# A fused attention and two-MLP kernel: nine slots with two MLP units, a third raw weight buffer, and another release for the low halves

## The reference

```python
scores = scale * q @ k.T                       # per batch and head, 576 x 576
kth = 32nd largest of each row
attn = softmax(where(scores >= kth, scores, -1e9))
x = attn @ v                                   # (4, 576, 512)
u = x + real(fft(fft(x, axis=1), axis=2))      # over tokens, then over width
u = u + relu(norm(u) @ w_ch1) @ w_ch2          # first MLP, norm without gain
out = u + relu((norm(u) * g_ln) @ w_ch1b) @ w_ch2b   # second MLP
```

## Time and profile before

| | us |
|---|---|
| median of 3 runs | 1462.12 |
| lowest to highest | 1460.74 to 1468.54 |
| the profiled execution | 1469.69 |
| its span, first to last instruction | 1467.9 |
| PE busy | 1299.5 (89%) |
| DVE busy | 1173.1 (80%) |
| ACT busy | 765.2 (52%) |
| POOL busy | 339.4 (23%) |

### The profile page before, as it was taken

The page is one execution under the profiler, slowest core; times in us unless marked ns, Lnnn a source line. Parts: engine busy times, 40 slices in busy tenths (PEclk is TensorE's granted clock), DMA queues, the critical chain, the costliest instruction groups (busy, mean ns, idle before and its releaser), DMA issues.

```text
span 1467.9 us, 22757 instructions
## 1 busy us (share of the span) xinstructions
PE 1299.5 (89%) x7944; PEld 1050.6 (72%) x7944; DVE 1173.1 (80%) x2332; ACT 765.2 (52%) x1480; POOL 339.4 (23%) x296
## 2 busy tenths in 40 slices
PE   4777778799989789778989988989999999999999
PEld 2444444577767677667877767877788999989898
DVE  8999999779999998899898899953675454555554
ACT  4666664466666554465563555542345344444433
POOL 3433330112122251122152132230113030121210
PEclk7878778899999889899998989999999999999999
DMA  6888892365646655666664656632344343333342
GB/s 228 292 308 311 290 341 88 131 230 197 225 155 218 228 193 177 218 219 224 240 204 152 214 199 221 215 127 98 101 158 158 129 138 128 126 119 125 119 149 82
DMA packets 113939, 274.34 MB, mean 187 GB/s; under 512 B 29345, under 2 KB 29346, under 8 KB 113826
## 3 DMA queue, kind: packets, MB, share of 16 engines
q1 hardware_dynamic: 102066, 225.68, 44.9%
q10 hardware_dynamic: 10368, 42.47, 8.3%
q0 software_dynamic: 1392, 4.73, 1.0%
HBM read 229.58 MB, written 42.73 MB: 186 GB/s over the span
## 4 chain that ended last, share of the span: by engine, by line
PE 51%; DVE 31%; DMA 6%; issue 5%; ACT 3%; POOL 3%; SPq 0%; ACTq 0%; DVEq 0%; POOLq 0%
PE Big L695 21%; DVE top L1041 13%; DVE wk L1053 12%; PE Big L678 11%; PE Sp L678 7%; DMA wf<-in_weights 6%; DVE ex L1060 3%; PE Tp L649 2%; PE Sp L722 2%; PE Tp L626 2%; DVE nmx L1048 2%; PE Sp L734 1%; PE Tp L643 1%; POOL un L497 1%; PE Tp L753 1%
## 5 line engine op out<-in xcount | busy, mean ns | idle before, releaser
L695 PE MATMUL Big<-wr,hh 128*128 128x512 f32 x1152 | 366.6, 400 | 0.0
L678 PE MATMUL Big<-uh,wr 128*128 128x256 f32 (+1 forms) x1336 | 305.9, 319 | 19.0 <-ACT hh L910 17.2
L1041 DVE MAX8 top<-wk 128x8 f32<-128x576 f32 x432 | 304.2, 744 | 0.0
L678 PEld LDWEIGHTS Big<-uh,wr 128*128 128x128 f32 x1336 | 225.8, 193 | 39.7 <-issue 29.1
L695 PEld LDWEIGHTS Big<-wr,hh 128*128 128x128 f32 x1152 | 220.5, 191 | 42.3
L695 PE MATMUL Big<-wr,hl 128*128 128x512 f32 x576 | 240.3, 417 | 4.6 <-DVE wr L1192 4.4
L1053 DVE MATCH_REPLACE8 wk<-top,wk 128x576 f32<-128x576 f32 x288 | 211.3, 740 | 0.0
L462 POOL TENSOR_TENSOR hl<-hf,hh 128x256 fp32r<-128x256 f32 (+1 forms) x111 | 93.3, 841 | 505.8 <-ACT hh L910 505.8
L678 PE MATMUL Big<-ul,wr 128*128 128x256 f32 (+1 forms) x668 | 208.3, 312 | 0.0
L626 PE MATMUL Tp<-ident,ex 128*128 128x128 f32 x720 | 121.6, 299 | 63.9 <-DVE ex L1060 59.7
L626 PEld LDWEIGHTS Tp<-ident,ex 128*128 128x128 f32 x720 | 90.0, 151 | 110.2 <-issue 78.2
(11 more groups left out here) (134 smaller groups left out, 1944.0 us busy)
## 6 DMA issues: line engine op xcount, KB each, us to landing
wf<-in_weights SPq DMA_DIRECT2D x200, 512.0 KB, 4.3
wr<-w_low SPq DMA_DIRECT2D x222, 256.0 KB, 4.1
sc<-in_weights SPq DMA_DIRECT2D x56, 512.0 KB, 3.2
sc<-sc_ahead ACTq DMA_DIRECT2D x36, 576.0 KB, 5.8
w_low<-wr SPq DMA_DIRECT2D x32, 512.0 KB, 6.8
sc_ahead<-U ACTq DMA_DIRECT2D x18, 576.0 KB, 5.5
sc_ahead<-un ACTq DMA_DIRECT2D x9, 576.0 KB, 3.1
sc_ahead<-yb ACTq DMA_DIRECT2D x9, 576.0 KB, 6.4
```

Of the source, the lines that this page charges most:

```text
L678: last = nc.tensor.matmul(hidden(n), a[:, kd * P:(kd + 1) * P], x[:, kd, 0:P * SIZE[p]], start=(kd == 0 and j == 0), stop=(kd == KD - 1 an ...
L695: last = nc.tensor.matmul(Ac[:, j, :], a[:, n % 2, j * P:(j + 1) * P], w, start=(f == 0 and m == 0), stop=(f == KF - 1 and m == 2))
L1041: nc.vector.max(top[:, s % RING, r, :], src).then_inc(s_top, 1)
```

## The change

- `DOUBLE` names nine slots (86, 92, 98, 104, 110, 121, 126, 132, 138) which carry two units. `UP` becomes 120, the list ends at slot 249, and the groups from the fifth on start earlier: 95, 109, 123, 137, 152, 168, ... in place of 97, 113, 129, 145, 161, 177, ...
- In such a slot the second unit stands last: PE runs its first layer and the first unit's second layer after `values_back`, ACT its relu and `highs` after `x_back`, POOL its low half near the end.
- The raw buffer `wf` has three parts (`WFS`), in the splitting stage and for units below `UP`.
- `weights_low` waits for even tiles on the negated maxima of the next pair, where it waited for the masks of the pair before.
- In every slot from 40 on ACT's `highs` stands behind `x_out`, ahead of the end-of-group copy and `x_back`.
- `ready_pair` and `rstd_slot` are adapted so that the group that starts at 152 is normalised in the last pair.

```diff
...
 RAWS = 4
+WFS = 3
 AHEAD = NT
...
 FIRST = NT + 3
+DOUBLE = (86, 92, 98, 104, 110, 121, 126, 132, 138)
+def planned():
+    slots, s = [FIRST] * BURST, FIRST + 1
+    while len(slots) < NUNITS:
+        slots += [s, s] if s in DOUBLE else [s]
+        s += 1
+    return slots
+SLOT_OF = planned()
...
-    return FIRST + max(n - BURST + 1, 0)
+    return SLOT_OF[n]
...
+def second_at(s):
+    return units_at(s)[1:] if s in DOUBLE else []
 def position(mlp, k):
...
-    return (START[p] - 6) // 2 if ORDER[p][0] == 1 else (START[p] - 5) // 2
+    n = (START[p] - 6) // 2 if ORDER[p][0] == 1 else (START[p] - 5) // 2
+    return min(n, PAIRS - 1) if START[p] < TILES + 12 else n
...
-    if START[p] >= TILES + 8:
+    if ready_pair(p) >= PAIRS:
         return START[p] - 10
...
         neghalf = sb("neghalf", [P, GC])
-        wf = sb("wf", [P, 2, 2, DM])
+        wf = sb("wf", [P, WFS, 2, DM])
         wr = sb("wr", [P, WRING, 2, 2, DM], f32r)
...
-            return n % 2 if n < UP else (n - UP) % RAWS
+            return n % WFS if n < UP else (n - UP) % RAWS
...
             r = raw_buffer(n)
-            if r < 2:
+            if r < 2 or n < UP:
                 return wf[:, r, :, :]
...
-            first = KF if raw_buffer(n) < 2 else 0
-            return 16 * (first + sum(raw_buffer(m) == raw_buffer(n) for m in range(n + 1)))
+            split = sum(j % WFS == raw_buffer(n) for j in range(2 * KF))
+            return 16 * (split + sum(raw_buffer(m) == raw_buffer(n) for m in range(n + 1)))
...
             load_ahead(0)
-            for j in range(2):
+            for j in range(WFS):
                 sp.dma_start(wf[:, j, :, :], w_raw[j]).then_inc(s_wraw[j], 16)
...
                 sp.wait_ge(s_wlow, j + 1)
-                if j + 2 < 2 * KF:
-                    sp.dma_start(wf[:, j % 2, :, :], w_raw[j + 2]).then_inc(s_wraw[j % 2], 16)
+                if j + WFS < 2 * KF:
+                    sp.dma_start(wf[:, j % WFS, :, :], w_raw[j + WFS]).then_inc(s_wraw[j % WFS], 16)
                 sp.dma_start(w_low[j], wr[:, j % WRING, :, 1, :].bitcast(f32)).then_inc(s_wst[j % WRING], 16)
...
                 r = n % WRING
-                if n >= 2:
-                    sp.wait_ge(s_w2h, n - 1)
+                if n >= WFS:
+                    sp.wait_ge(s_w2h, n - WFS + 1)
                 sp.dma_start(raw(n), w_raw[tile_index(n)]).then_inc(s_wraw[raw_buffer(n)], 16)
...
                 if j % 2 == 0:
-                    pool.wait_ge(s_masked, j + 2)
+                    pool.wait_ge(s_negmax, j // 2 + 2)
                 pool.wait_ge(s_whigh, j + 1)
                 r = j % WRING
-                pool.tensor_tensor(wr[:, r, :, 1, :], wf[:, j % 2, :, :], wr[:, r, :, 0, :].bitcast(f32),
+                pool.tensor_tensor(wr[:, r, :, 1, :], wf[:, j % WFS, :, :], wr[:, r, :, 0, :].bitcast(f32),
                                    ALU.subtract).then_inc(s_wlow, 1)
...
                 for n in units_at(s):
-                    if n < UP:
+                    if n < UP and n not in second_at(s):
                         unit(n)
...
                         gain(p, s - (START[p] - 5))
+                for n in second_at(s):
+                    unit(n)
                 if s < TILES and s % NT == LAST_SHARED + 2:
...
                     for n in units:
-                        mlp1(n)
+                        if n not in second_at(s):
+                            mlp1(n)
                     for t in turns_at(s):
...
                     values_back(s)
+                for n in second_at(s):
+                    mlp1(n)
+                    mlp2(n - 1)
                 if 0 < s <= AHEAD:
...
             def weights_high(j):
-                act.wait_ge(s_wraw[j % 2], 16 * (j // 2 + 1))
+                act.wait_ge(s_wraw[j % WFS], 16 * (j // WFS + 1))
                 if j >= WRING:
                     act.wait_ge(s_wst[j % WRING], 16 * (j // WRING))
-                nc.scalar.activation(wr[:, j % WRING, :, 0, :], wf[:, j % 2, :, :], ACT.Copy).then_inc(s_whigh, 1)
+                nc.scalar.activation(wr[:, j % WRING, :, 0, :], wf[:, j % WFS, :, :], ACT.Copy).then_inc(s_whigh, 1)
...
                     for n in units_at(s):
+                        if n in second_at(s):
+                            continue
                         relu_out(n)
...
                     x_out(s)
+                if s != START[0]:
+                    for n in units_at(s):
+                        if n not in second_at(s):
+                            highs(n)
                 for n in closing_at(s):
...
                     x_back(s)
+                for n in second_at(s):
+                    relu_out(n)
+                    highs(n)
                 if s % 2 == 1 and s + 1 < 2 * KF:
...
                 for n in units_at(s):
-                    if s != START[0]:
-                        highs(n)
                     if UP <= n + 2 < NUNITS:
```

## The result

| | kernel before | changed kernel |
|---|---|---|
| median, us | 1461.63 (4 runs, 1460.74 to 1468.54) | 1441.09 (4 runs, 1436.72 to 1443.21) |
| ratio to before, 95% interval | | 0.9842 [0.9808, 0.9876] |
| profiled execution, us | 1469.69 | 1436.72 |
| its span | 1467.9 | 1434.8 |

The changed kernel is 1.6% faster. The forecast was 1436, range 1410 to 1457. The two profiled executions lie 33.0 us apart and the medians 20.5: the profile of before is slower than any of its four runs, that of after is the fastest of its four.

The account below looks back on a forecast made before the run. Attention was taken as paced by DVE's top-32 search with PE close behind, the MLP part as all PE. Terms -14 - 3 + 25 - 34 = -26 gave span 1442, run 1444 and median 1436 us, range 1410 to 1457.

Parts of the forecast that it names:

- low halves behind the maxima: First stretch: POOL's even low half starts after DVE's negation, which falls from 1.09 to 0.17 us in 16 pairs: -14 us.
- third buffer and early copies: Raw loads leave SP 0.65 us earlier, counting at perhaps five of the 31 waits on the path: -3 us.
- nine doubles, attention: Attention slots 86 to 143: nine slots carry a second unit, partly hidden in PE's idle: +25 us.
- nine doubles, tail: MLP tail: nine units fewer at 4.17 us, -37.5, less 3.5 lost at the last batch's combines: -34 us.
- The bandwidth doubt: First stretch: HBM bandwidth binds, pairs stay near 12.2 us and the low halves gain little: 1450 us, chance 0.12.
- The rival that the doubles hide: Attention: PE's idle time takes in the doubled slots' work, +8 us instead of +25: 1419 us, chance 0.22.
- the one that they cost their full work: Attention: doubles cost +39 us and the earlier load gains nothing: 1453 us, chance 0.10.
- The load-bound rival: Doubled slots: the second high copy waits a whole 7.1 us load in each of nine, +64 us: 1478 us, chance 0.06.
- The +3.5 at the combines: Tail: the last batch's DFT combines meet two-tile units, so DVE's work outlasts PE's in two slots: +3.5 us.
- a fuller PE is granted the upper level more often: Attention: an argument for the doubles hiding, a busier PE gets 2.4 GHz more often; mean clocks 0.92, 0.89, 0.95.

Follow-up runs that it names:

- e2: Changed kernel with POOL's even low halves released by the masks again, as in the kernel before: 1454.5 us.
- e9: Kernel before with one edit, POOL's even low halves wait for the negated maxima: 1454.3 us.
- e1: Changed kernel with DOUBLE empty, so one unit in every slot from 40 on: 1443.1 us.
- e4: Changed kernel with SP's raw load issued ahead of its wait for a second layer: 1420.3 us.
- e6: Changed kernel without doubles and with ACT's high copies at the end of the slot again: 1438.8 us.
- e3: Changed kernel with two raw buffers in place of three: 1437.5 us.
- e7: Changed kernel without doubles and with two raw buffers: 1442.2 us.
- e11: Changed kernel with only three doubles, in slots 86, 92 and 121: 1431.3 us.

## Why the prediction was right

| step | forecast | measured |
|---|---|---|
| low halves behind the maxima | -14 | -14.8 in the negations (17.50 to 2.71), 15 by pair 17; -13.4 (e2) and -11.6 (e9) in medians |
| third buffer and early copies | -3 | -9.4 at the tail's start (955.4 to 946.0), -11.2 in medians (e9 to e1; -9.4 against their own runs of the kernel before) |
| nine doubles, attention | +25 | +34.0 (e1 to changed) |
| nine doubles, tail | -34 | -39.1 |
| sum | -26 | -20.5 in medians, -33.1 between the spans of the two profiles |

The total is right within 6 us on the median (1436 against 1441) and within 7 on the span of the profile (1442 against 1434.8). Only the first term is right in its mechanism and its size. The other three were each off by 5 to 9 us, two one way and one the other, so the closeness of the sum is in part luck. The doubles as a whole were to gain 9 us and gained 2.0 by the medians and 5.1 by the profiles.

*Low halves.* Every part came as worked out: which instruction, its 0.92 us, 16 times. The Trainium skill (SBUF — State Buffer, SBUF: two separate sides) says that whoever starts first on the shared port keeps it for the whole instruction; e2 and e9 agree, since the wait comes and goes with POOL's start alone. The bandwidth doubt is answered: the stretch moved 314 GB/s, and the pair from 120.8 moved 387 with DVE busy 11.27 of 11.30 us:

```profile
120.80:132.10 11.30, 6.83 (x57) 4.24 (x56) 11.27 (x26) 8.14 (x12) 4.71 (x2) 1.00 1.05 387
```

That is above the figure of about 358 GB/s which the Trainium skill (SBUF — State Buffer, A bandwidth-pool intuition that's wrong) gives for HBM, and which so was no ceiling over one pair.

*Third buffer.* The step was worked out rightly for one load: it leaves 0.64 us earlier (median 1.00 to 0.36), held from then on by SP's wait for a second layer, and e4 shows that this wait is what keeps ACT waiting. The term was mis-sized, -3 for -9 to -11. What failed is the count: the prediction let 0.65 us count at five of the 31 waits, and more must have counted. With the copies last and three buffers ACT's waits fall from 56.8 to 26.7 us, and the buffer alone gains 13.2 to 15.5 us (e9 to e6), with SP's order as it was. So that order doesn't make the buffer worthless. In the changed kernel it is worthless (e3, and e7 against e1) because the early copies had freed the load already, and they cost 4.3 us beside it. How 0.64 us a load, 42 us in sum, becomes 13 to 16 at the end was not followed through.

*The doubles.* The six with three-tile units were priced 18 and cost 26.7 to 27.7: the prediction let PE's idle in the level stretches absorb a third of their work, and it absorbed nothing. Slots 86, 92 and 121 were priced 7 and cost 6.3 to 8.8, but not where they were to: in e11 86 was to cost 3 and cost 3.8, 92 was to be hidden and cost 3.8, and 121 was to cost 4 and had added 0.7 by slot 128. There two errors cancelled. In slot 86 the price was to come from DVE's mask standing 7 us, and it stood 4.50. The rival that the doubles hide is refuted; the one that they cost their full work describes all nine in the attention (6 x 4.37 + 3 x 3.0 = 35.2 us of work, 35.5 from slot 86 on). The load-bound rival is refuted: ACT did wait twice, but for loads of 4 to 4.7 us beside PE's own work, and e4, which cut those waits, made the doubles cheaper by 5 us at most.

*The tail.* The units gave their 37.5 us. The +3.5 at the combines became one stop of 4.75 us and 7.6 in all, and almost half of the stop is a collision with POOL that wasn't in the working. Not foreseen either was the 4.6 us that the new starts of the groups took away from `pair_x`. Some 4.6 us of the 39.1 aren't traced to a place. Both places show the mechanism of the first term: the prediction looked for DVE instructions slowed by POOL in the first stretch, and there were more in the tail.

## What to carry to other kernels

Before adding a buffer or moving a load, list every wait that stands ahead of the load in its queue, and which of them ends last. Here there were two gates. The first could be opened in two ways that didn't add, a third buffer (13 to 16 us) or earlier copies (10 to 12), and the second by moving one load ahead of one wait (13 us without doubles, 20.8 with them). Moving work under a stage pays only if the stage's engine has time for it where it lands: no double was hidden, six of the nine cost more than they gave back (10 us by the medians), and the other three gained mostly by where they moved the starts of the groups. And start the slow partner of a shared port after the short instruction that it would hold up, in every stage: after each change of the plan look again for DVE instructions that take longer than their like.

## What the runs showed of the hardware

The granted clock reads 0.95 at its upper level in the profile of the kernel before and 1.00 in that of after (steady tails in the earlier trace rows and above), yet a first layer takes 2.09 us in both. Here a change of that reading is no change of speed, and the mean clocks of two profiles (0.907 and 0.945 for the same kernel, spans 1467.9 and 1468.6) say little of their times.

A stop of PE costs more than its own length. After the 4.75 us in the changed kernel the clock reads 0.50, the lower of its two levels, from 1043 to 1048 us, and a two-tile first layer takes 2.56 us where it takes 1.42 at the upper level.

An f32 tensor_tensor on DVE takes 1.1 us longer beside POOL's f32 additions in both places (2.32 us and not 1.22 for `pair_x`, 1.52 and not 0.42 for the combine), and POOL's three additions take 5.22 us there and 3.73 in e11, where they meet no `pair_x`.

That a fuller PE is granted the upper level more often, as a rival of the prediction says, doesn't come out of its rows: 0.92 with PE busy 85% of the stretch, 0.89 with 88%, 0.95 with 93%.
